# Two attention-fed MLP layers on one core: slots of the first pass reordered, two pairs of batches interleaved by tiles in the third, sums on GpSimd

## What is computed

```python
a = exp(phi - max(phi, axis=2)); a = a / (sum(a, axis=2) + 1e-09)
k_m = einsum('bhsm,bhsd->bhmd', a, k); v_m = einsum('bhsm,bhsd->bhmd', a, v)
scores = (q @ k_m.T) / 8; attn = softmax over m (with + 1e-09 in the divisor)
x = (attn @ v_m) as (4608, 512)
h = x @ w_in;  g = where(h > 0, h, exp(min(h, 0)) - 1);  x = g @ w_out      # first MLP
h = x @ w_in;  g = h * clip(h + 3, 0, 6) / 6;            out = g @ w_out    # second MLP
```

## Time and profile before

| | us |
|---|---|
| median of 3 runs | 1660.97 |
| lowest, highest | 1654.18, 1663.56 |
| profiled execution, its own time | 1659.14 |
| its span, first to last instruction | 1657.4 |
| TensorE busy | 1521.6 (92%) |
| DVE busy | 1102.4 (67%) |
| ScalarE busy | 729.4 (44%) |
| GpSimd busy | 264.9 (16%) |

### The profile page before, as it was taken

One profiled execution on the slowest core, in us unless ns is written; L12 is line 12 of the kernel. 1 busy time (PEld: TensorE's weight loads), 2 busy tenths in 40 slices (PEclk: granted clock), 3 DMA queues, 4 the chain that ended last, 5 costly groups with the idle time before them and its releaser, 6 DMA issues.

```text
span 1657.4 us, 30358 instructions
## 1 busy us (share of the span) xinstructions
PE 1521.6 (92%) x12080; PEld 1433.1 (86%) x12080; DVE 1102.4 (67%) x1528; ACT 729.4 (44%) x1037; POOL 264.9 (16%) x278
## 2 busy tenths in 40 slices
PE   6788988888979999999997999999986999999998
PEld 4576767676769999999996999999986999999998
DVE  4656666666557888888854666677656577777775
ACT  2456665756643444444433334444332333333333
POOL 0325333434100000000001233344310000000000
PEclk9789999999989999999998999999998999999999
DMA  9477779787685555555567445544579333333330
GB/s 251 129 212 228 241 238 287 252 247 241 226 304 183 186 183 183 183 183 183 178 226 283 164 164 180 179 154 151 186 270 338 129 128 127 129 129 130 130 130 34
DMA packets 209213, 318.26 MB, mean 192 GB/s; under 512 B 9456, under 2 KB 140528, under 8 KB 209136
## 3 DMA queue, kind: packets, MB, share of 16 engines
q1 hardware_dynamic: 199088, 285.81, 52.2%
q10 hardware_dynamic: 10048, 31.43, 5.4%
HBM read 178.78 MB, written 138.41 MB: 191 GB/s over the span
## 4 chain that ended last, share of the span: by engine, by line
PE 69%; DVE 12%; DMA 8%; ACT 7%; issue 3%; POOL 0%; SPq 0%; ACTq 0%; DVEq 0%
PE ps L435 22%; PE ps L437 21%; PE ps L436 21%; DMA layer_hidden<-eg 3%; PE ps L491 2%; ACT e L764 2%; DMA rows_a<-in_phi 2%; DVE g L1053 2%; ACT e L766 2%; DVE ga_lo L1267 1%; DVE w_lo L1044 1%; DMA kv<-in_v 1%; PE ps L515 1%; ACT ga_hi L918 1%; PE ps L458 1%
## 5 line engine op out<-in xcount | busy, mean ns | idle before, releaser
L435 PE MATMUL ps<-xc_hi,tile 128*128 128x288 f32 x896 | 271.9, 303 | 41.6 <-DVE c_sum L1201 37.9
L435 PE MATMUL ps<-tile,ga_lo 128*128 128x256 f32 x1008 | 289.5, 287 | 13.6 <-DVE ga_lo L1267 13.1
L435 PE MATMUL ps<-ring_hi,tile 128*128 128x256 f32 x1008 | 287.6, 285 | 3.7 <-DMA tile<-forms_out 3.7
L437 PE MATMUL ps<-tile,ga_hi 128*128 128x256 f32 x1008 | 287.4, 285 | 0.0
L436 PE MATMUL ps<-tile,ga_hi 128*128 128x256 f32 x1008 | 287.4, 285 | 0.0
L436 PE MATMUL ps<-ring_lo,tile 128*128 128x256 f32 x1008 | 286.7, 284 | 0.0
L437 PE MATMUL ps<-ring_hi,tile 128*128 128x256 f32 x1008 | 286.6, 284 | 0.0
L436 PE MATMUL ps<-xc_lo,tile 128*128 128x288 f32 x896 | 269.3, 301 | 0.0
L437 PE MATMUL ps<-xc_hi,tile 128*128 128x288 f32 x896 | 268.3, 299 | 0.0
L435 PEld LDWEIGHTS ps<-xc_hi,tile 128*128 128x128 f32 x896 | 172.8, 193 | 45.0 <-DVE c_sum L1201 40.4
L435 PEld LDWEIGHTS ps<-tile,ga_lo 128*128 128x128 f32 x1008 | 195.3, 194 | 17.2 <-issue 11.9
(11 more groups left out here) (178 smaller groups left out, 2778.1 us busy)
## 6 DMA issues: line engine op xcount, KB each, us to landing
layer_hidden<-g SPq DMA_DIRECT2D x128, 288.0 KB, 3.1
x<-layer_hidden SPq DMA_DIRECT2D x36, 1024.0 KB, 5.2
layer_hidden<-eg SPq DMA_DIRECT2D x64, 576.0 KB, 3.0
a<-layer_hidden SPq DMA_DIRECT2D x36, 1024.0 KB, 7.5
forms_out<-forms_a SPq DMA_DIRECT2D x20, 896.0 KB, 4.9
tile<-forms_out SPq DMA_DIRECT2D x8, 1792.0 KB, 8.6
forms_in<-forms_b SPq DMA_DIRECT2D x16, 896.0 KB, 5.6
tile<-forms_in ACTq DMA_DIRECT2D x8, 1792.0 KB, 13.7
```

The costliest lines, as they stand in the source:

```text
L435: nc.tensor.matmul(dst, a_lo, b_hi, start=first, stop=False, skip_group_check=onto)
L437: return nc.tensor.matmul(dst, a_hi, b_hi, start=False, stop=last, skip_group_check=onto)
```

## The change

1. **Slots.** `SLOT` and `SHORT` replace the four tables. In a group's eight steps, before: Q0 PHI | Q1 MAX | SC | SUB | EXP SUM | NORM | KV | PT KMT. Now: Q0 PHI | MAX Q1 | SUB SC | EXP SUM | NORM KV | KMT | PT | nothing. (PHI, MAX, SUB, SUM, KV and KMT are those of the next group.) The short groups of the first 12 steps stay as they were. Pieces move by one step.
2. **Sums.** `xc_sums` for batches 1 to 7 goes from the DVE to GpSimd, where it stands behind the first `right_sums` of a batch.
3. **First pair.** Batches 0 and 1 take turns: tiles 0 to 3 of batch 0, 0 to 3 of batch 1, 4 to 7 of batch 0, 4 to 7 of batch 1. Tile loads 4 to 7 start in steps 4 to 7. The columns of batch 1 are wanted in step 4, cast in steps 1 to 3. The columns of batch 2 are loaded in step 12 of the pair instead of behind step 7, and cast in steps 13 and 14. SyncE no longer waits for the first layer's stores before batch 0.
4. **Last pair.** Batches 6 and 7 take turns as `LAST_PAIR` says; `used_up` loads a tile of the fourth pass as soon as batch 7 has used the old one. The quads a11, a21, a22 are issued in step 61, behind its predecessor's store, instead of at the start of batch 7. The addition a21 + a22 moves to the last step, a11 - a21 into the fourth pass.

```diff
-        QUERIES = {0: (S_Q0,), 1: (S_Q1,), 2: (S_SC,), 4: (S_EXP,), 5: (S_NORM,), 7: (S_PT,)}
-        VALUES = {0: (S_PHI,), 1: (S_MAX,), 3: (S_SUB,), 4: (S_SUM,), 6: (S_KV,), 7: (S_KMT,)}
...
+        SLOT = {0: ((S_Q0, 0), (S_PHI, 1)), 1: ((S_MAX, 1), (S_Q1, 0)), 2: ((S_SUB, 1), (S_SC, 0)), 3: ((S_EXP, 0), (S_SUM, 1)),
+                4: ((S_NORM, 0), (S_KV, 1)), 5: ((S_KMT, 1),), 6: ((S_PT, 0),)}
...
-        PIECE_LOADS = {0: 0, 3: 1, 9: 2}
-        PIECE_SUMS = {2: 0, 5: 1, 11: 2}
-        PIECE_STORES = {4: 0, 7: 1, 14: 2}
+        PIECE_LOADS = {0: 0, 2: 1, 8: 2}
+        PIECE_SUMS = {2: 0, 4: 1, 10: 2}
+        PIECE_STORES = {5: 0, 7: 1, 13: 2}
...
+        FIRST_PAIR = [(0, f) for f in range(4)] + [(1, f) for f in range(4)] + [(0, f) for f in range(4, FH)] + [(1, f) for f in range(4, FH)]
+        LAST_PAIR = [(B - 2, f) for f in range(5)] + [(B - 1, f) for f in range(5)] + \
+            [(B - 2, 5), (B - 2, 6), (B - 1, 5), (B - 2, 7), (B - 1, 6), (B - 1, 7)]
...
+        def rows_at(u):
+            if isinstance(u, int) and u in (0, B - 2):
+                return {1: (0,), 2: (1, 2), 3: (3,)}
+            if isinstance(u, int) and u == 1:
+                return {5: (0, 1), 6: (2, 3)}
+            return {3: (0,), 4: (1,), 5: (2,), 6: (3,)}
...
+            def used_up(at):
...
+                f = LAST_PAIR[at][1]
+                act.wait_ge(up_done[3], STEPS2 - 2 * FH + at + 1)
...
+                load_tile(2, f)
...
                     if not first or f > 0:
                         up_three(u * FH + f - 1, (f - 1) % FH)
                     up_c11(u, f)
-                    if not last and 3 <= f < 7:
-                        xc_split_hi(u + 1, 1 - buf, f - 3)
...
+                    for n in () if last else rows_at(u).get(f, ()):
+                        xc_split_hi(u + 1, 1 - buf, n)
...
-                    if not last and f == 2:
-                        xc_sums(u + 1, 1 - buf)
-                    if last and f == 4:
+                    if last and f == FH - 1:
                         s1_s3(0, 0, 1)
...
+                    if isinstance(u, int) and u == 1 and f == 4:
+                        load_xc(2, 0)
                     if follows and f == FH - 1:
                         load_xc(u + 2, buf)
                     store_g(u, f)
...
+                    if isinstance(u, int) and u == B - 1 and f == 5:
+                        sp.wait_ge(stage_c.stored, 16 * 2 * (FH - 2))
+                        load_quad(a11, 0, 0, 0, a11_loaded)
+
+                        sp.wait_ge(up_done[3], STEPS2 - 2 * FH + LAST_PAIR.index((B - 2, FH - 1)) + 1)
+                        load_quad(a21, 0, 1, 0, a21_loaded)
+                        load_quad(a22, 0, 1, 1, a22_loaded)
```

More of the change, by code:

```diff
@@ L632, in up_block @@
                 first = isinstance(u, int) and u == 0
[L633 to L637 removed]
+                for i in range(FH):
+                    n, (batch, f), rows = u * FH + i, step_of(u, i), buffer_of(u, i, buf)
+                    if f == 0 and not (isinstance(batch, int) and batch == 0):
+                        pe.wait_ge(xc_ready, 4 * (batch + 1))
+                    if isinstance(batch, int) and batch == 0 and f > 1:
                         pe.wait_ge(tile_loaded[f], 32)
[L639 to L641 removed]
+                    up_open(n, f, rows, i)
+                    if i > 0:
+                        up_close(n - 1, step_of(u, i - 1)[1], buffer_of(u, i - 1, buf), i - 1)
                     elif not first:
[L643 to L644 removed]
+                        up_close(n - 1, step_of(u - 1, FH - 1)[1], buffer_of(u - 1, FH - 1, 1 - buf), FH - 1)
+                    up_middle(n, f, rows, i)
             def down_grain(i, q):
@@ L877, in up_block @@
                     up_first(u, f)
[L878 removed]
+                    if first:
                         if f == 1:
                             act.wait_ge(xg_used, GRAINS * BLOCKS)
[L881 removed]
+                        if f == 0 or f > 3:
+                            load_tile(1, max(f, 3))
                     if not first or f > 0:
@@ L1282, in down_block @@
                     grain_split_lo(i, parity, q)
+                    if first and q == 1:
+                        s1_s3(0, 0, 3)
                     if q == 1:
@@ L1427, in up_block @@
                 makes = not isinstance(u, int) or u > 0
-                if makes:
-                    right_sums(stage_c, 2 * (u - 1))
-                    piece_lo(stage_c, 2 * (u - 1))
-                for n in range(2):
-                    xc_split_lo(u + 1, 1 - buf, n)
-                if makes:
-                    right_sums(stage_c, 2 * (u - 1) + 1)
-                for n in range(2, 4):
-                    xc_split_lo(u + 1, 1 - buf, n)
-                if makes:
-                    piece_lo(stage_c, 2 * (u - 1) + 1)
+                early, late = isinstance(u, int) and u in (0, B - 2), isinstance(u, int) and u == 1
+                k = 2 * (u - 1)
+                if early:
+                    xc_sums(u + 1, 1 - buf)
+                    for n in range(4):
+                        xc_split_lo(u + 1, 1 - buf, n)
+                if makes:
+                    right_sums(stage_c, k)
+                    if not early and not late:
+                        xc_sums(u + 1, 1 - buf)
+                    piece_lo(stage_c, k)
+                    if not early and not late:
+                        for n in range(2):
+                            xc_split_lo(u + 1, 1 - buf, n)
+                    right_sums(stage_c, k + 1)
+                    if late:
+                        xc_sums(u + 1, 1 - buf)
+                    if not early:
+                        for n in range(0 if late else 2, 4):
+                            xc_split_lo(u + 1, 1 - buf, n)
+                    piece_lo(stage_c, k + 1)
             nc.gpsimd.memset(ident[:], 1.0).then_inc(ident_made, 1)
@@ L1680, in _ @@
             up_block(B - 2, 0, follows=False)
-            sp.wait_ge(stage_c.stored, 16 * 2 * (FH - 2))
-            sp.wait_ge(up_done[3], STEPS2 - FH)
-            load_quad(a21, 0, 1, 0, a21_loaded)
-            load_quad(a22, 0, 1, 1, a22_loaded)
-            load_quad(a11, 0, 0, 0, a11_loaded)
             up_block(B - 1, 1, makes=False, follows=False)
```

98 lines of the change are left out of this document (58 added, 40 removed).

## The result

| | before | changed |
|---|---|---|
| median of 18 runs, us | 1656.96 | 1671.66 |
| lowest, highest | 1649.76, 1664.79 | 1656.87, 1682.44 |
| profiled execution, its own time | 1659.14 | 1660.51 |
| its span | 1657.4 | 1658.8 |

The changed kernel is slower by 0.8%: ratio 1.0076, 95% interval 1.0052 to 1.0099, where 1627 us was forecast. It also spreads wider, over 25.6 us instead of 15.0 (20.8 without the 1682.44, which counts as a slow execution and is left out of the ratio), and its profiled execution is one of its quickest, so the two traces differ by only 1.4 us.

The account below looks back on a forecast made before the run. TensorE was taken to set the time, so only its waits could be won. Slots -25, sums -20, first pair -1 and +7.7, last pair -8.5 and +13.3 give -33.5 us: 1627 us from the median 1660.97, range 1602 to 1646.

Parts of the forecast that it names:

- the whole 25: First pass, new slots: 35.7 us of TensorE waits go, about 11 us of new ones come, net -25 us.

Follow-up runs that it names:

- experiments 4: The changed kernel with the first pass's tile loads still in step 8, but phi, keys and values loaded in step 10: 1658.6 us (ratio 1.0009).
- 3: The changed kernel with the weight tiles of batches 2 to 5 of the first pass loaded in step 10 instead of 8: 1640.9 us (0.9884).

## What to carry to other kernels

When a stage moves, list what its stage issues on each DMA queue and add up the bytes ahead of the next transfer that an engine waits for. Where a large load stands was right, if at all, for the old order only. A number in an order table is not a time: look for what an engine really waits for before you move work by it. And where one instruction is sometimes seven times as long as its median, find what runs beside it before you put it first in anyone's path. When a fix helps the changed kernel, give it to the kernel before as well: the tile's move was worth 11.4 us there, and without that run the whole 25 would have gone to the slots.

## What the runs showed of the hardware

- **The DVE held by GpSimd.** A maximum of 96x128 took 0.29 us alone and 2.04 to 2.13 us beside GpSimd's 128x896 addition, and ended within 0.15 us of it in both kernels: a block until the end and no sharing. The Trainium skill says so (SBUF — State Buffer, section on the two separate sides): a DVE instruction with both inputs in SBUF and a GpSimd instruction that reads SBUF take the shared ports in turn, and whichever comes second waits for the whole of the other. The trace agrees. The DVE's instructions of the third pass with one input in PSUM did not lengthen beside 9.3 us of low halves (0.46 us for u3 throughout).
- **A transfer lands behind what its queue holds.** A gate store of 288 KB landed in 2.2 us with nothing ahead of it, in 6.5 to 8.7 us behind one tile load (experiments 4 and 3), and in 12.9 us behind 4.7 MB issued in the 7.2 us before it. The tile issued at 213.04 landed at 227.0, the store behind it at 227.8. The Trainium skill, DMA: Bandwidth & Descriptors, section on queues, rings and completion order, has descriptors of a ring taken in order; these landings agree.
- **A stall costs more than its wait.** A wait of 4.4 us on the DVE, 3.5 on TensorE, made a group 6.8 us longer, with the granted clock at 0.77 over the 15 us behind it.
